# Attention windows with two expert layers on one core: opening order, input split by blocks, four weight stages

## The chip, the cores and the metric

One NeuronCore of a Trainium2 chip runs one program. The time is the device time of one execution in microseconds (us), lower is better. Engines: TensorE (PE), VectorE (DVE), ScalarE (ACT), GpSimd (POOL), and SyncE (SP), which issues every DMA of this kernel.

## The reference

Inputs r, k, v, w, a, b have the shape (4, 8, 768, 40), all float32. The recurrence over 768 tokens is, for each of 32 heads:

```
y[t]  = r[t] @ state
Sa    = state @ a[t]
state = state * w[t] - outer(Sa, b[t]) + outer(v[t], k[t])
```

y becomes x of (3072, 320). Then `h = ((x @ w1) * (x @ w2)) @ w3`, `x2 = h @ w_out`, with inner size 1024; then `g = max(x2 @ w_in, 0)`, `out = (g * g) @ w_out2`, with inner size 2048.

## The kernel before

**Attention.** The sequence is cut into 24 windows (n = 0 to 23) of 64 tokens of two batches. Each window goes through a fixed chain of steps on PE: `turn_w`, `turn_ar`, `turn_bk` (transposes of inputs), `cross`, `turn_rows`, `make_z`, then `make_u0`, `make_x1`, `make_u1` (a solve by blocks with inverted 32x32 blocks), `turn_uv`, `add_state`, `make_read`, `make_y`, `turn_state`. ACT and DVE stand between them: `scan`, `invert_decay`, `scale_a`, `scale_bk`, `mask_ak`, `fill_lanes`, `turn_inverse`, `add_x1`, `new_state`, `mask_read`, `scale_y` on DVE; `copy_r`, `copy_blocks`, `copy_rows`, `copy_x`, `reset`, `copy_u`, `copy_uvT`, `place_state`, `copy_state` on ACT. POOL computes the inverses (`invert`, L650 to L660): 31 steps of one multiplication and one addition per window, each step after the last; `turn_inverse(n)` on DVE hands the result to `make_u0(n)`. `store_y(n)` on SP writes y, transposed, to DRAM.

**Fold.** w3 @ w_out is multiplied out first, in eight row blocks `ft`: the block of w3 is loaded into a stage (`load_staged(ft)`), turned (`turn_w3`, PE), copied (`copy_w3`, ACT), multiplied in four quarters (`multiply_w3(ft, part)`, PE), split into a rounded high part and a rest (`round_fold` on ACT, `rest_of_fold` on DVE) and stored (`store_fold`, SP).

**Experts.** All large products run in a 4-byte type of lower precision, each operand being split in such a high part and a rest. The tokens go through in six tiles of 512; tile i needs windows 4i to 4i + 3, and `load_x`, `round_x` (ACT, the cast into `xT_hi`) and `rest_x` (DVE, `xT_lo`) bring its input. x has 320 rows, kept as three blocks of 128 (the last holds 64 rows twice, once for each of high part and rest). `into_hidden` (L854) multiplies a tile by one slice of w1, w2 or w_in with eight matmuls; `fold` (L907) and `project` (L922) multiply back. In the first tile each weight slice is split on the fly: SP loads it to a stage (`load_staged`), `round_split` (ACT) and `rest_of_split` (DVE) write it to a ring, `store_split` (SP) saves it to DRAM; later tiles load it from there. `splits` lists these slices in the order of their slots. There are LOOK = 3 stages; split x uses stage (8 + x) modulo 3, and `pass_split(x)` on SP stores split x and then loads x + 3.

**Order.** Each engine's program is a list written out by hand; semaphores connect the lists, and an engine does nothing past a step that waits. The opening is a flat list of steps: windows 0 to 3, the first part of windows 4 and 5, and the whole fold. Then come windows 4 to 23, whose steps are laced with those of the experts: after each step, `next(beside)` lets a generator do one piece of the experts. The first of these that PE does is `into_hidden("a0")` of tile 0, and `make_u0(4)` stands right behind it. Windows 0 to 3 use two PSUM areas (`both` for even n, `aside` for odd n), later ones `both` alone.

The lines that set the pace in what follows (before `make_u0`, and `turn_inverse` on DVE):

```
def make_u0(n):
    pe.wait_ge(inverse_turned, n + 1)
    pe.wait_ge(x_copied, n + 1)
    if n < OPENING - 1:
        pe.wait_ge(masked_ak, 2 * (n + 3))
        pe.wait_ge(blocks_copied, 2 * (n + 3))
```

Of the kernel before, what the change touches and what calls it, by code (L numbers as in the profile page):

```python
# [5 lines left out]
F32 = mybir.dt.float32  # L6
F32R = mybir.dt.float32r
ALU = mybir.AluOpType
# [69 lines left out]
def attention_with_experts(nc, xT_dram, inputs, w1, w2, w3, w_out, w_in, w_out2, out):  # L78
# [8 lines left out]
    T, M = out.shape  # L87
# [15 lines left out]
    LOOK = 3  # L103
# [10 lines left out]
    with ExitStack() as ctx:  # L114
# [33 lines left out]
        stage = [sb(f"stage{x}", [P, STAGE]) for x in range(LOOK)]  # L148
# [159 lines left out]

        staged_count = []
        for x in range(FT + len(splits)):  # L310
            before = staged_count[x - LOOK] if x >= LOOK else 0
            staged_count.append(before + 16 * (1 if x < FT or splits[x - FT][1] else 6))
# [9 lines left out]
        def staged_w(x):  # L322
            return stage[(FT + x) % LOOK][:, 0:2 * DX].rearrange("p (n c) -> p n c", n=2)

# [11 lines left out]
        def _(sp):  # L336
# [15 lines left out]
            def load_x(i, h):  # L352
                tile = xT_dram.rearrange("k (b s) -> k b s", b=B)[:, 2 * h:2 * h + 2, 2 * C * i:2 * C * (i + 1)]
                wait(sp, x_split, i)
# [15 lines left out]
            def load_staged(x):  # L370
                signal = staged[x % LOOK]
                if x < FT:
                    sp.dma_start(stage[x % LOOK][:], w3[x * P:(x + 1) * P, :]).then_inc(signal, 16)
                    return
                _, kind, at = splits[x - FT]
                if kind:
                    sp.dma_start(stage[x % LOOK][:, 0:M], w_out2[(at - FT) * P:(at - FT + 1) * P, :]).then_inc(signal, 16)
                    return
                for n in range(2):
# [5 lines left out]
                    for row in (0, REM):  # L385
                        sp.dma_start(dst[row:row + REM, 2 * P:DX], src[2 * P:M, lo:lo + P]).then_inc(signal, 16)
# [159 lines left out]
            next_staged(6)  # L546
            next_uv(2)
            next_ar(4)
            store_fold(2)
            next_staged(7)  # L550
            store_fold(3)
            store_y(0)
            next_bk(4)
            next_zv(4)
            next_w(5)
            next_uv(3)
            next_staged(8)
            next_ar(5)
            store_fold(4)
            store_y(1)  # L560
            next_bk(5)
            next_staged(9)
# [3 lines left out]
            store_fold(5)  # L566
            store_y(2)
            pass_split(0)
            load_x(0, 0)
            pass_split(1)  # L570
            store_y(3)
            load_x(0, 1)
            next_staged(10)
            store_fold(6)
# [96 lines left out]
        def _(pe):  # L671
# [198 lines left out]
            def turn_w3(ft):  # L870
                pe.wait_ge(staged[ft % LOOK], staged_count[ft])
                for part in range(PARTS):
                    u = PARTS * ft + part
                    wait(pe, w3_copied, u - 1)
                    for x in range(4):
                        g = 4 * part + x
                        last = nc.tensor.transpose(turning(u)[:, x * P:(x + 1) * P],
                                                   stage[ft % LOOK][:, g * P:(g + 1) * P], ident[:])
# [50 lines left out]
            def experts():  # L929
# [4 lines left out]
                for i in range(TILES):  # L934
# [6 lines left out]
                    pe.wait_ge(x_split, i + 1)  # L941
                    for f in range(FT + LAG):
                        if f < FT:
                            at = (FT + FT2 // 2) * i + f
                            wait_w(at)
                            for n, use in enumerate((f"a{f}", f"b{f}")):
                                wait_bank(pe, use, i)
                                into_hidden(use, w_ring[at % SLOTS], 5 * P * n, xT_hi, xT_lo)
# [66 lines left out]
            make_u0(1)  # L1015
            multiply_w3(4, 0)
            make_y(0)
            turn_state(0)
            make_x1(1)
            turn_rows(2)  # L1020
            multiply_w3(4, 1)
            make_u1(1)
            make_z(2)
            turn_uv(1)
            turn_w(4)
            multiply_w3(4, 2)
            add_state(1)
            turn_ar(4)
            multiply_w3(4, 3)
            make_read(1)  # L1030
            turn_bk(4)
            turn_w3(5)
# [4 lines left out]
            multiply_w3(5, 0)  # L1037
# [3 lines left out]
            make_x1(2)  # L1041
            multiply_w3(5, 1)
            turn_w3(6)
            make_u1(2)
            multiply_w3(5, 2)
            turn_uv(2)
            multiply_w3(5, 3)
            add_state(2)
            make_u0(3)
            make_read(2)  # L1050
            make_x1(3)
            make_y(2)
            turn_state(2)
            make_u1(3)
            turn_rows(4)
            turn_uv(3)
            make_z(4)
            add_state(3)
            multiply_w3(6, 0)
            make_read(3)  # L1060
            multiply_w3(6, 1)
            make_y(3)
            turn_state(3)
            multiply_w3(6, 2)
            turn_ar(5)
            multiply_w3(6, 3)
            turn_w3(7)
            turn_bk(5)
            multiply_w3(7, 0)
            cross(5)  # L1070
            multiply_w3(7, 1)
            multiply_w3(7, 2)
            multiply_w3(7, 3)
# [42 lines left out]
        def _(act):  # L1116
# [71 lines left out]
            def round_split(x):  # L1188
                _, kind, at = splits[x]
                act.wait_ge(staged[(FT + x) % LOOK], staged_count[FT + x])  # L1190
                if kind:
                    wait_slot_v(act, at)
                    nc.scalar.copy(v_ring[at % SLOTS][:, 0:M], stage[(FT + x) % LOOK][:, 0:M]).then_inc(v_rounded, 1)
# [24 lines left out]
            def round_x(i):  # L1218
# [3 lines left out]
                nc.scalar.copy(xT_hi[:], x_raw[:]).then_inc(x_rounded, 1)  # L1222
# [78 lines left out]
            place_state(0)  # L1301
            copy_u(1, 0, u0_made, u0_copied)
            copy_state(0)
            copy_rows(2)
            copy_u(1, 1, u1_made, u1_copied)
            copy_x(2)
            reset(2)
            copy_uvT(1)
            copy_r(4)
            place_state(1)  # L1310
            round_fold(4)
            copy_w3(5)
            copy_state(1)
            copy_blocks(4)
            copy_rows(3)
            copy_u(2, 0, u0_made, u0_copied)
            copy_x(3)
            reset(3)
            round_split(0)
            copy_w3(6)  # L1320
            copy_u(2, 1, u1_made, u1_copied)
            copy_uvT(2)
            round_fold(5)
            round_split(1)
            copy_u(3, 0, u0_made, u0_copied)
            place_state(2)
            copy_state(2)
            copy_u(3, 1, u1_made, u1_copied)
            copy_rows(4)
            copy_uvT(3)  # L1330
            copy_x(4)
# [3 lines left out]
            round_fold(6)  # L1335
            copy_w3(7)
            round_x(0)
            round_fold(7)
# [370 lines left out]
```

## Time and profile before

| | us |
|---|---|
| median of 3 runs | 1100.56 (1098.77 to 1101.25) |
| the profiled execution | 1100.62 |
| its span, first to last instruction | 1098.1 |
| PE busy | 1052.2 (96%) |
| DVE busy | 634.2 (58%) |
| ACT busy | 415.1 (38%) |
| POOL busy | 553.1 (50%) |

Mean granted clock of TensorE 0.984 of full speed. Busy time counts instructions on the engine, not DMA issues or waits. An engine that is idle is no loss by itself: it counts where the chain of work that ends last passes through it. DMA moved 172.74 MB.

### The profile page before, as it was taken

The numbers are of one execution on the slowest core, as the hardware profiler recorded it, in microseconds if no ns is written. First come the engines' busy times: TensorE is split into PE (matmuls) and PEld (weight loads), VectorE is DVE, ScalarE is ACT, GpSimd is POOL, SyncE is SP. The second block draws the span as 40 slices with busy tenths as digits, with TensorE's granted clock in tenths as the row PEclk, the third lists the DMA queues.
The fourth block names the chain that finished last, engine by engine and source line by source line (L and its number), as shares of the span: only waits on it lengthen the run. The fifth ranks groups of instructions, "written<-read, shape, count | busy, mean of one in ns | idle before, by whom it ended". The sixth has DMA issues, their size and how long they took to land.

```text
span 1098.1 us, 27872 instructions
## 1 busy us (share of the span) xinstructions
PE 1052.2 (96%) x11056; PEld 895.0 (81%) x11056; DVE 634.2 (58%) x987; ACT 415.1 (38%) x771; POOL 553.1 (50%) x1573
## 2 busy tenths in 40 slices
PE   6989689999989999999999999999999999999998
PEld 5767678778868888888888888888888888898897
DVE  7848256677757556656546657556566556333333
ACT  3444234344434234334234334224334234332232
POOL 4778727537555364585374575473675463600000
PEclk9999699999999999999999999999999999999999
DMA  9944367666768646647645658645557543546552
GB/s 169 190 101 92 84 182 201 157 170 188 190 201 229 148 135 150 151 147 196 158 138 136 151 154 204 156 130 141 148 160 202 146 136 103 156 144 227 180 166 76
DMA packets 269504, 172.74 MB, mean 157 GB/s; under 512 B 201792, under 2 KB 231488, under 8 KB 269376
## 3 DMA queue, kind: packets, MB, share of 16 engines
q1 hardware_dynamic: 269376, 170.97, 59.9%
q8 instruction: 88, 1.44, 0.6%
q14 instruction: 40, 0.33, 0.1%
HBM read 144.18 MB, written 26.74 MB: 156 GB/s over the span
## 4 chain that ended last, share of the span: by engine, by line
PE 77%; DVE 3%; issue 2%; SPq 2%; ACT 1%; DMA 0%; DVEq 0%; ACTq 0%
PE aside L854 30%; PE moe_bank L922 15%; PE moe_bank L907 9%; PE both L816 3%; PE both L717 3%; PE both L758 2%; PE both L750 2%; PE both L831 2%; PE both L827 2%; PE both L799 2%; PE both L701 1%; PE both L730 1%; PE both L840 1%; PE both L781 1%; PE both L807 1%
## 5 line engine op out<-in xcount | busy, mean ns | idle before, releaser
L656 POOL TENSOR_TENSOR inv_tmp<-blk,inv 128x60 f32<-128x60 f32 (+24 forms) x744 | 244.4, 328 | 252.2 <-DVE blk L1428 195.2
L660 POOL TENSOR_TENSOR inv<-inv,inv_tmp 128x60 f32<-128x60 f32 (+24 forms) x744 | 265.6, 357 | 58.3
L922 PE MATMUL moe_bank<-v_ring,h_hi 128*128 128x320 f32 x768 | 178.7, 320 | 0.0
L1508 DVE TENSOR_TENSOR hidden<-left 128x512 f32<-128x512 f32 x96 | 67.9, 707 | 129.6 <-ACT left L1216 129.6
L854 PE MATMUL aside<-xT_hi,w_ring 128*128 128x512 f32 x480 | 132.8, 406 | 0.1
L854 PE MATMUL aside<-x2T_hi,w_ring 128*128 128x512 f32 x480 | 132.7, 406 | 0.0
L922 PEld LDWEIGHTS moe_bank<-v_ring,h_hi 128*128 128x128 f32 x768 | 128.2, 190 | 3.3
L1496 DVE TENSOR_TENSOR h_lo<-hidden,h_hi 128x512 fp32r<-128x512 f32 x144 | 99.0, 688 | 48.1 <-ACT h_hi L1204 47.5
L1216 ACT ACTIVATE left<-aside 128x512 f32<-128x512 f32 x96 | 57.3, 597 | 172.2 <-PE aside L854 102.6
L922 PE MATMUL moe_bank<-v_ring,h_lo 128*128 128x320 f32 x384 | 119.2, 310 | 0.0
L1204 ACT CAST h_hi<-hidden 128x512 fp32r<-128x512 f32 x144 | 89.5, 621 | 77.0 <-DVE hidden L1504 38.4
L854 PEld LDWEIGHTS aside<-xT_hi,w_ring 128*128 128x128 f32 x480 | 84.5, 188 | 16.6 <-DVE xT_lo L1513 0.3
L854 PEld LDWEIGHTS aside<-x2T_hi,w_ring 128*128 128x128 f32 x480 | 84.1, 188 | 15.0 <-ACT x2T_hi L1242 0.2
L907 PE MATMUL moe_bank<-h_hi,v_ring 128*128 128x512 f32 x288 | 93.3, 405 | 0.0
L1386 DVE RECIPROCAL undecay<-decay 104x256 f32<-104x256 f32 x48 | 83.6, 1743 | 0.3
L854 PE MATMUL aside<-xT_lo,w_ring 128*128 128x512 f32 x288 | 81.5, 391 | 0.0
L854 PE MATMUL aside<-x2T_lo,w_ring 128*128 128x512 f32 x288 | 81.4, 391 | 0.0
L1504 DVE TENSOR_TENSOR hidden<-left,aside 128x512 f32<-128x512 f32 x48 | 32.8, 682 | 70.9 <-PE aside L854 70.9
L922 PEld LDWEIGHTS moe_bank<-v_ring,h_lo 128*128 128x128 f32 x384 | 72.8, 190 | 0.0
L854 PEld LDWEIGHTS aside<-x2T_lo,w_ring 128*128 128x128 f32 x288 | 54.1, 188 | 12.3 <-DVE x2T_lo L1532 0.2
L854 PEld LDWEIGHTS aside<-xT_lo,w_ring 128*128 128x128 f32 x288 | 54.1, 188 | 11.9
L1151 ACT COPY uv<-both 32x320 f32<-32x320 f32 x88 | 36.7, 417 | 62.2 <-PE both L758 60.8
(146 smaller groups left out, 1605.3 us busy)
## 6 DMA issues: line engine op xcount, KB each, us to landing
w_ring<-gate_rows SPq DMA_DIRECT2D x40, 640.0 KB, 4.6
w_ring<-win_rows SPq DMA_DIRECT2D x40, 640.0 KB, 4.1
v_ring<-wout_rows SPq DMA_DIRECT2D x80, 320.0 KB, 3.0
v_ring<-fold_rows SPq DMA_DIRECT2D x48, 384.0 KB, 4.1
gate_rows<-w_ring SPq DMA_DIRECT2D x8, 640.0 KB, 3.8
win_rows<-w_ring SPq DMA_DIRECT2D x8, 640.0 KB, 4.1
wout_rows<-v_ring SPq DMA_DIRECT2D x16, 320.0 KB, 2.8
stage<-in_moe_w SPq DMA_DIRECT2D x8, 512.0 KB, 4.9
```

The source lines that it names most:

```text
L656: nc.gpsimd.tensor_tensor(tmp, x[:, j, 0:j].unsqueeze(2).broadcast_to([P, j, X - lo]), mine[:, j:j + 1, lo:X].broadcast_to([P, j, X - lo]) ...
L660: nc.gpsimd.tensor_tensor(mine[:, 0:j, lo:X], mine[:, 0:j, lo:X], tmp, ALU.add).then_inc(solve, 1)
L717: last = nc.tensor.matmul(its_both(n)[:, x * P:(x + 1) * P], bkT[n % 2][0:E, x].rearrange("e z s -> e (z s)"), azk[n % 2][0:E, x].rearrang ...
L854: last = nc.tensor.matmul(bank(use), w, x, start=n == 0, stop=n == len(terms) - 1)
L907: last = nc.tensor.matmul(bank(f"x{m}"), weights[:, lo:lo + P], h[at % RING][:], start=f == 0 and n == 0, stop=f == FT - 1 and n == 2)
L922: last = nc.tensor.matmul(bank(f"o{s}")[:, 0:M], h[at % RING][:, s * P:(s + 1) * P], weights[:, rest * M:(rest + 1) * M], start=f == 0 and ...
L1151: last = nc.scalar.copy(uv[n % 2][rows, :, q, 0:D], by_head(its_first(n), rows))
L1204: nc.scalar.copy(h_hi[at % RING][:], hidden[x % 2][:]).then_inc(hi_made, 1)
L1216: drain(nc.scalar.activation(left[x % 2][:], bank(use), ACT.Relu), use)
L1386: nc.vector.reciprocal(undecay[0:E, xs], decay[n % 4][0:E, xs, 1:C + 1]).then_inc(undecayed, 1)
L1496: nc.vector.tensor_tensor(h_lo[at % RING][:], hidden[x % 2][:], h_hi[at % RING][:].bitcast(F32), ALU.subtract).then_inc(lo_made, 1)
L1508: nc.vector.tensor_tensor(hidden[x % 2][:], left[x % 2][:], left[x % 2][:], ALU.mult).then_inc(squared, 1)
```

## The change

Three things. First, `LOOK` is 4: a fourth stage, only as large as a weight slice. w3's blocks go on using the stages 0 to 2; the slices use 3, 2, 0, 1 in turn. `pass_split(x)` loads x + 4, and the opening loads four slices (8 to 11) by `next_staged`. The last 64 rows of a slice, which go to the stage twice, are loaded by one DMA whose source is repeated, where there were two DMAs; a slice thus takes four DMAs, not six.

Second, `round_x` and `rest_x` do a tile's input in three blocks, and the matmuls of `into_hidden("a0")` wait for the block that each reads, not for the whole.

Third, the lists of the opening are laid out anew on all engines but POOL. Nothing is added or left out.

```diff
-    LOOK = 3
+    LOOK = 4
-        stage = [sb(f"stage{x}", [P, STAGE]) for x in range(LOOK)]
+        stage = [sb(f"stage{x}", [P, STAGE if x < LOOK - 1 else 2 * DX]) for x in range(LOOK)]
...
+        def stage_of(x):
+            return x % (LOOK - 1) if x < FT else (3, 2, 0, 1)[(x - FT) % LOOK]
...
-                    for row in (0, REM):
-                        sp.dma_start(dst[row:row + REM, 2 * P:DX], src[2 * P:M, lo:lo + P]).then_inc(signal, 16)
+                    twice = src[2 * P:M, lo:lo + P].unsqueeze(0).broadcast_to([2, REM, P])
+                    sp.dma_start(dst[:, 2 * P:DX], twice).then_inc(signal, 16)
...
             def next_staged(x):
-                sp.wait_ge(turned_w3, PARTS * (x - LOOK + 1))
+                before = [y for y in range(min(x, FT)) if stage_of(y) == stage_of(x)]
+                wait(sp, turned_w3, PARTS * (before[-1] + 1) if before else 0)
...
-                    pe.wait_ge(x_split, i + 1)
+                    def wait_x(n):
+                        if n in (0, 2, 4):
+                            pe.wait_ge(x_rounded, 3 * i + n // 2 + 1)
+                        elif n > 4:
+                            pe.wait_ge(x_split, 3 * i + n - 4)
...
-                nc.scalar.copy(xT_hi[:], x_raw[:]).then_inc(x_rounded, 1)
+                for k in range(3):
+                    nc.scalar.copy(xT_hi[:, k], x_raw[:, k]).then_inc(x_rounded, 1)
...
-                dve.wait_ge(x_rounded, i + 1)
-                nc.vector.tensor_tensor(xT_lo[:], x_raw[:], xT_hi[:].bitcast(F32), ALU.subtract).then_inc(x_split, 1)
+                for k in range(3):
+                    dve.wait_ge(x_rounded, 3 * i + k + 1)
+                    nc.vector.tensor_tensor(xT_lo[:, k], x_raw[:, k], xT_hi[:, k].bitcast(F32),
+                                            ALU.subtract).then_inc(x_split, 1)
```

The new lists from `turn_w3(4)` on (m(ft, part) is `multiply_w3`):

```
PE    turn_w3(4) make_read(0) m(4,0) turn_w3(5) make_y(0) turn_state(0) make_u0(1) turn_rows(2) make_x1(1)
      make_z(2) turn_w(4) make_u1(1) m(4,1) turn_uv(1) turn_ar(4) add_state(1) m(4,2) make_read(1) turn_bk(4)
      make_y(1) turn_state(1) cross(4) turn_rows(3) m(4,3) make_u0(2) turn_w(5) make_z(3) make_x1(2) m(5,0)
      make_u1(2) m(5,1) turn_uv(2) m(5,2) add_state(2) m(5,3) make_read(2) turn_w3(6) make_y(2) turn_state(2)
      m(6,0) turn_rows(4) m(6,1) make_u0(3) make_z(4) make_x1(3) m(6,2) make_u1(3) m(6,3) turn_uv(3)
      turn_w3(7) add_state(3) m(7,0) make_read(3) m(7,1) make_y(3) turn_state(3) m(7,2) turn_ar(5) m(7,3)
      turn_bk(5) cross(5)
ACT   copy_w3(4) place_state(0) copy_w3(5) copy_state(0) copy_u(1,0) copy_rows(2) round_split(0) copy_x(2)
      reset(2) copy_u(1,1) copy_uvT(1) copy_r(4) place_state(1) copy_state(1) copy_blocks(4) copy_rows(3)
      round_fold(4) copy_u(2,0) copy_x(3) reset(3) copy_u(2,1) copy_uvT(2) place_state(2) round_fold(5)
      copy_w3(6) copy_state(2) copy_rows(4) copy_u(3,0) round_split(1) copy_x(4) copy_u(3,1) round_fold(6)
      copy_uvT(3) copy_w3(7) place_state(3) copy_state(3) copy_r(5) round_fold(7) round_x(0)
DVE   new_state(0) rest_of_fold(3) mask_read(0) turn_inverse(1) fill_lanes(3) scale_y(0) add_x1(1)
      rest_of_split(0) scan(4) invert_decay(4,0) invert_decay(4,1) new_state(1) scale_a(4) mask_read(1)
      scale_bk(4) scale_y(1) turn_inverse(2) mask_ak(4) fill_lanes(4) scan(5) add_x1(2) rest_of_fold(4)
      invert_decay(5,0) invert_decay(5,1) new_state(2) rest_of_fold(5) mask_read(2) scale_y(2)
      turn_inverse(3) add_x1(3) rest_of_split(1) rest_of_fold(6) new_state(3) mask_read(3) scale_y(3)
      scale_a(5) rest_of_fold(7) scale_bk(5) rest_x(0)
```

The old list of PE in the same part, where it differs most: `... turn_w3(4) make_read(0) make_u0(1) m(4,0) make_y(0) ...`, then `... m(5,3) add_state(2) make_u0(3) make_read(2) make_x1(3) make_y(2) turn_state(2) make_u1(3) turn_rows(4) turn_uv(3) make_z(4) add_state(3) m(6,0) make_read(3) m(6,1) make_y(3) turn_state(3) m(6,2) turn_ar(5) m(6,3) turn_w3(7) turn_bk(5) m(7,0) cross(5) m(7,1) m(7,2) m(7,3)`.

## Rows read from the trace of the kernel before

**Rows 1.** The page's 40 slices: PE's busy tenths and its clock in tenths.
```profile
PE   6989689999989999999999999999999999999998
PEclk9999699999999999999999999999999999999999
```

**Rows 2.** Timeline of PE, 0 to 200 us: start, duration, instructions, [idle before, releaser].
```profile
69.24 1.06 PE L758 MATMUL aside<-x_row,invT 32*32 32x40 f32 x32 [3.73 <-DVE invT L1434]
...
97.74 0.76 PE L758 MATMUL both<-x_row,invT 32*32 32x40 f32 x32 [0.76 <-DVE azk L1419]
98.43 0.65 PE L685 MATMUL both<-ident,w_raw 64*104 64x64 f32 x8
...
107.28 1.24 PE L889 MATMUL moe_bank<-wo_raw,hidden 128*128 128x320 f32 x4
108.54 0.81 PE L807 MATMUL both<-uv,bk_row 128*40 128x40 f32 x32
118.21 1.28 PE L758 MATMUL aside<-x_row,invT 32*32 32x40 f32 x32 [8.85 <-DVE invT L1434]
...
135.13 0.81 PE L807 MATMUL aside<-uv,bk_row 128*40 128x40 f32 x32
...
137.05 1.95 PE L816 MATMUL aside<-rbd,uvT 104*128 104x128 f32 x16
...
149.46 2.05 PE L717 MATMUL both<-azk,bkT 104*128 104x128 f32 x16 [0.24 <-DVE bkT L1407]
...
158.95 0.76 PE L758 MATMUL both<-x_row,invT 32*32 32x40 f32 x32 [2.28 <-DVE azk L1419]
```

**Rows 3.** Waits of PE, 160 us to the end: total, times, longest; first of five.
```profile
PE both L799 <- DVE decay L1378: 5.2, 1, 5.2
...
```

**Rows 4.** Timeline of POOL: copies that start inverses, and one long step.
```profile
68.43 0.40 POOL L650 COPY inv<-inv_unit 128x256 f32<-128x256 f32 x1
...
91.97 0.40 POOL L650 COPY inv<-inv_unit 128x256 f32<-128x256 f32 x1
...
103.85 2.26 POOL L656 TENSOR_TENSOR inv_tmp<-blk,inv 128x64 f32<-128x64 f32 x1
...
117.39 0.40 POOL L650 COPY inv<-inv_unit 128x256 f32<-128x256 f32 x1
```

**Rows 5.** Stretches of PE: from:to, length, busy (count), granted clock, DMA share, GB/s.
```profile
128.00:131.00 3.00, 3.00 (x72) 0.50 0.20 45
...
310.00:312.00 2.00, 2.00 (x11) 0.53 0.92 327
```

**Rows 6.** Timeline of DVE, 0 to 215 us.
```profile
96.08 1.41 DVE L1419 TENSOR_TENSOR azk<-both,above 64x512 f32<-64x512 f32 x2
...
103.67 1.75 DVE L1386 RECIPROCAL undecay<-decay 104x256 f32<-104x256 f32 x1
105.34 0.63 DVE L1488 TENSOR_TENSOR w_ring<-stage,w_ring 128x512 fp32r<-128x512 f32 x1
...
142.48 0.69 DVE L1470 TENSOR_TENSOR y_out<-aside,decay 104x512 f32<-104x512 f32 x1 [2.22 <-PE aside L831]
...
152.57 1.76 DVE L1513 TENSOR_TENSOR xT_lo<-x_raw,xT_hi 128x1536 fp32r<-128x1536 f32 x1 [3.17 <-ACT xT_hi L1222]
...
155.65 0.73 DVE L1434 STREAM_TRANSPOSE invT<-inv 128x256 f32<-128x256 f32 x1
```

**Rows 7.** Timeline of ACT, at 151 and at 305 us.
```profile
151.07 1.47 ACT L1222 CAST xT_hi<-x_raw 128x1536 fp32r<-128x1536 f32 x1 [3.07 <-DMA x_raw<-xT]
...
304.68 0.83 ACT L1196 CAST w_ring<-stage 128x768 fp32r<-128x768 f32 x1 [4.86 <-DMA stage<-in_moe_w_in]
```

**Rows 8.** Timeline of SP's DMA issues, 268 to 330 us.
```profile
287.81 0.62 SPq L399 DMA_DIRECT2D wout_rows<-v_ring  x1
...
296.14 0.47 SPq L383 DMA_DIRECT2D stage<-in_moe_w_in  x1
```

**Rows 9.** DMA queue, 104.6 to 109.3 us, one slice's load: packets, MB, share.
```profile
q1 hardware_dynamic: 784, 0.36, 27.2%
```

More of the change, by code:

```diff
@@ L307, in due @@
             return [x for x, (slot, _, _) in enumerate(splits) if x >= EARLY and slot == t - LEAD]
+        def stage_of(x):
+            return x % (LOOK - 1) if x < FT else (3, 2, 0, 1)[(x - FT) % LOOK]
         staged_count = []
         for x in range(FT + len(splits)):
-            before = staged_count[x - LOOK] if x >= LOOK else 0
-            staged_count.append(before + 16 * (1 if x < FT or splits[x - FT][1] else 6))
+            counted = [staged_count[y] for y in range(x) if stage_of(y) == stage_of(x)]
+            staged_count.append((counted or [0])[-1] + 16 * (1 if x < FT or splits[x - FT][1] else 4))
         clears = [azk[0], rbd[0], azk[1], rbd[1], *spare, *zv, *sT, *st]
@@ L1014, in _ @@
             make_read(0)
-            make_u0(1)
             multiply_w3(4, 0)
+            turn_w3(5)
             make_y(0)
             turn_state(0)
+            make_u0(1)
+            turn_rows(2)
             make_x1(1)
-            turn_rows(2)
+            make_z(2)
+            turn_w(4)
+            make_u1(1)
             multiply_w3(4, 1)
-            make_u1(1)
-            make_z(2)
             turn_uv(1)
-            turn_w(4)
+            turn_ar(4)
+            add_state(1)
             multiply_w3(4, 2)
-            add_state(1)
-            turn_ar(4)
-            multiply_w3(4, 3)
             make_read(1)
             turn_bk(4)
-            turn_w3(5)
             make_y(1)
@@ L1036, in _ @@
             turn_rows(3)
-            multiply_w3(5, 0)
+            multiply_w3(4, 3)
             make_u0(2)
@@ L1041, in _ @@
             make_x1(2)
+            multiply_w3(5, 0)
+            make_u1(2)
             multiply_w3(5, 1)
-            turn_w3(6)
[L1044 to L1051, printed above, removed]
+            turn_uv(2)
+            multiply_w3(5, 2)
+            add_state(2)
+            multiply_w3(5, 3)
+            make_read(2)
+            turn_w3(6)
             make_y(2)
             turn_state(2)
+            multiply_w3(6, 0)
+            turn_rows(4)
+            multiply_w3(6, 1)
+            make_u0(3)
+            make_z(4)
+            make_x1(3)
+            multiply_w3(6, 2)
             make_u1(3)
-            turn_rows(4)
+            multiply_w3(6, 3)
             turn_uv(3)
-            make_z(4)
+            turn_w3(7)
             add_state(3)
-            multiply_w3(6, 0)
+            multiply_w3(7, 0)
             make_read(3)
-            multiply_w3(6, 1)
+            multiply_w3(7, 1)
             make_y(3)
             turn_state(3)
-            multiply_w3(6, 2)
+            multiply_w3(7, 2)
             turn_ar(5)
-            multiply_w3(6, 3)
-            turn_w3(7)
+            multiply_w3(7, 3)
             turn_bk(5)
-            multiply_w3(7, 0)
             cross(5)
-            multiply_w3(7, 1)
-            multiply_w3(7, 2)
-            multiply_w3(7, 3)
             for n in range(OPENING, WINDOWS):
@@ L1315, in _ @@
             copy_rows(3)
+            round_fold(4)
             copy_u(2, 0, u0_made, u0_copied)
@@ L1602, in _ @@
             new_state(0)
+            rest_of_fold(3)
+            mask_read(0)
             turn_inverse(1)
             fill_lanes(3)
-            mask_read(0)
-            rest_of_fold(3)
             scale_y(0)
             add_x1(1)
+            rest_of_split(0)
             scan(4)
             invert_decay(4, 0)
+            invert_decay(4, 1)
             new_state(1)
             scale_a(4)
-            invert_decay(4, 1)
             mask_read(1)
             scale_bk(4)
+            scale_y(1)
             turn_inverse(2)
-            rest_of_fold(4)
-            scale_y(1)
             mask_ak(4)
@@ L1621, in _ @@
             scan(5)
+            add_x1(2)
+            rest_of_fold(4)
             invert_decay(5, 0)
-            add_x1(2)
             invert_decay(5, 1)
-            rest_of_split(0)
+            new_state(2)
             rest_of_fold(5)
-            new_state(2)
+            mask_read(2)
+            scale_y(2)
             turn_inverse(3)
+            add_x1(3)
             rest_of_split(1)
-            mask_read(2)
-            add_x1(3)
-            scale_y(2)
+            rest_of_fold(6)
             new_state(3)
```

70 lines of the change are left out of this document (35 added, 35 removed).

## The prediction

> **What bounds the kernel now.** I read the slices of the page first, then TensorE's order of time, then the list of its waits, and last the engines that those name. The slices [rows 1] show TensorE (PE) at 9 tenths nearly everywhere; the weak ones lie in the first 15% of the span, and the granted clock dips there too. Later PE is busy without pause. So a microsecond taken out of an early wait of PE comes off the end; one taken off another engine later is worth nothing. The waits of PE worth naming [rows 2, 3]: 3.73 us before `make_u0(1)` at 69.24, 8.85 us before `make_u0(3)` at 118.21, 2.28 us before `make_u0(4)` at 158.95, and one of 5.2 us in the experts' first tile (before `turn_uv`, at 309 us). The first two are waits for an inverse: POOL works on them back to back, one from 68.43 to 91.97 (23.54 us), the next to 117.39 (25.42) [rows 4]. During the 8.85 us PE still has `make_read(2)`, `make_y(2)`, `turn_state(2)` and the last two of W3's eight row blocks to do, but they stand behind `make_u0(3)` in its queue. After that wait the clock is low, 0.50 (1.2 GHz) still in 128 to 131 [rows 5]; `make_read(3)` at 137.05 takes 1.95 us again.
>
> **Opening, up to the third inverse.** The new order puts `turn_w3(5)`, `make_y(0)` and `turn_state(0)` ahead of `make_u0(1)`, so PE is busy on from 65.5 (69.24 - 3.73). From 69.24 to 97.74 the old order took 28.5 us [rows 2]; about 3.8 of it were small waits and low clock, and it had one quarter of a `multiply_w3` (1.24) more than the new one has there. That gives 65.5 + 28.5 - 3.8 - 1.2 = 89.0, and 90.5 with two waits that I find in the new order (`turn_rows(2)` for `scale_y(0)`, `turn_uv(1)` for `copy_u(1, 1)`, which has moved behind `reset(2)`). There PE waits: `make_u0(2)` needs `mask_ak(4)`, which is behind `turn_inverse(2)` on DVE, and this waits for POOL until 91.97: + 0.8 to turn it + 2.3 for the mask (1.41 [rows 6] and two copies) gives 95.0, against 97.74. The new wait, 4.5 us, holds up all that is behind it on PE, but not the path: from there to the end of `add_state(2)` the old order took 11.6 us (97.74 to 109.35 [rows 2]). With `make_read(2)` 1.95, its mask 1.2, `make_y(2)` 2.0, `turn_state(2)` 0.8, `turn_rows(4)` 0.9 and two quarters of W3 at 1.1 a piece, PE arrives at `make_u0(3)` at 115.7. The inverse is later still.
>
> **When inverse 3 ends.** Its 25.42 us hold one TENSOR_TENSOR of 2.26 us at 103.85 [rows 4], where its neighbours take 0.3. It ran beside DVE's reciprocal at 103.67, right behind which stood `rest_of_split(0)` (from 105.34 [rows 6]), and ended in the middle of that. The new order has no such pair there: `rest_of_split(0)` comes at some 74.5 us. So I take 23.5 us as for inverse 2, and 0.5 for what `rest_of_split(0)` now costs inverse 2: 91.97 + 0.5 + 23.5 = 116.0, and 0.82 on to `make_u0(3)` (117.39 to 118.21): **T0 = 116.9**. With a 2.26 us op again it is 118.9.
> The Trainium skill (SBUF — State Buffer, "SBUF: two separate sides") lets a DVE op with two SBUF inputs shut out POOL's reads, but names nothing by which a reciprocal would; by it the cause of the first 1.5 us is another and may stay, T0 would be 118.4 and the time 1082.9.
>
> **From T0 to the experts.** Window 2 shows the same chain at full clock: `make_u0` at 97.74 to `add_state` at 108.54, 10.80 us [rows 2]. The new one for window 3 lacks `turn_w` (0.6) and two quarters of W3 (2.3): 7.9. Then `add_state` to `make_read`, 1.92 (135.13 to 137.05); to the end of `scale_y(3)`, 6.12 (143.17 [rows 6]); y's way through DRAM to the cast of x, 7.90 (ACT at 151.07 [rows 7]). Sum: ACT begins `round_x(0)` at T0 + 23.8. PE's own way there, ending in `cross(5)`, ended 8.3 us after `scale_y(3)` before (149.46 + 2.05 = 151.51); now with one quarter of W3 less in front, 7.2: hidden by x, by little.
> Split by blocks: one cast of 1.47 and one subtraction of 1.76 [rows 6, 7] become three each, of 0.6 by estimate (a third, and 0.1 for an instruction more); a subtraction starts 0.65 after its cast, and the last ends 2.4 us after ACT began, against 3.26. PE may begin 0.65 us after ACT, not 3.5. But behind the eight matmuls of `a0` stands `make_u0(4)`, which needs `mask_ak(5)`, behind `rest_x(0)` on DVE: 3.30 us from `turn_inverse(4)` to it (155.65 to 158.95), and `rest_of_fold(7)` is gone from between them. So it comes at ACT + 5.7, where it was + 7.88. The split is worth 2.2 us, not the 2.9 that PE gains at the door; its wait before `make_u0(4)` grows from 2.28 to 2.8. In the five later tiles x is ready long before and no wait of PE is for it [rows 3], so it is worth 0 there, and the 0.3 us more on ACT and on DVE lie beside PE's matmuls.
> `make_u0(4)` at 116.9 + 23.8 + 5.7 = 146.4, was 158.95: **12.5 us**. With T0 = 118.9 it is 10.5, with 0.6 less of small waits 13.1.
>
> **Four stages, not three.** The 5.2 us at 309 go back so: `turn_uv` waits for DVE's scan; this stands behind `rest_of_split` of a w_in slice, and that behind ACT's cast, which sat idle 4.86 us until its stage had landed, at 304.68 [rows 7]. SP issued that load only from 296.14 on, six issues to 300.9. With four stages it goes out one split earlier, behind the store at 287.81 [rows 8], and with four issues is out at 291.5; landed at 294 to 297. ACT is free for it at 299.8. So the wait goes whole, and the scan's input (`turn_w`, done at 301.0) is no later than the old one's slot. It also takes the low clock behind it (0.53 in 310 to 312 [rows 5]): 3 us at half speed, 1.5. Together **6.7 us**, bounds 0 (late all the same) and 7.5. No other cast waits for a stage, so the other early loads bring 0, and two issues less of 0.57 us a slice only relieve SP.
> One DMA where two were: its source repeats 64 rows twice, the repeat outermost. In the old trace the 784 packets of one slice took 27.2% of 16 engines over 4.7 us [rows 9], 0.026 us each. Spread over 16 engines, nothing changes. Should only two engines carry the 128 packets, two such transfers a slice put 6.7 us on two engines together, 3.3 each if they share, up to 6.7 if not, and the slice lands 3 us later, at 297 to 300: still in time for 299.8. I take 6.7 either way.
> The Trainium skill speaks for the bad case (DMA: Bandwidth & Descriptors, "Rules for kernel authors": an outermost zero-stride dim of c copies confines the DMA to c engines); no row here shows which engine carries what.
>
> **Sum.** The profiled execution took 1100.6 (span 1098.1), the runs' median to 0.1. 1100.6 - 12.5 - 6.7 = **1081.4 us**; own range 1078 to 1085.
>
> **Rivals.**
> (a) The clock. After 8.85 us of waiting PE ran at half speed for some 15 us. If the 4.5 us before `make_u0(2)`, or the short waits around T0, bring that on in the tail, which holds some 15 us of PE's work, 7.5 us come back: 1088.9. For it: after the 3.73 us `make_u0(1)` took 1.06 for 0.76. Against: by the later rows this was over soon. 14%.
> (b) The stage's load is late again, SP's queue having shifted with all the rest: 1100.6 - 12.5 = 1088.1. Against: 3 to 5 us of margin. 9%.
> (c) The other side: two engines carry the repeated rows, and what is queued behind them on these (window inputs, ring loads) comes late. Twelve slices are loaded in the first tile, each with 2.9 us more (3.3 for 0.4) on either engine; if PE waits for all of it, 35 us: 1116. It turns the sign from 1.6 us a slice on (19.2 / 12). For it: DMA is half to nine tenths busy in that stretch. Against: no wait in [rows 3] is for a DMA. 4%.
> (d) The order stalls where I overlooked something and the two cancel, within 0.2% (2.2 us, what can be told from no change here): 3%.
> The forecast has 70%. Faster 0.94, same 0.03, slower 0.03 (a part of (c) only eats the gain). Range for 8 in 10: 1077 to 1088.5.
>
> **What would show it.** PE without a gap from 62 to 70; a wait of 4 to 5 us before `make_u0(2)` near 95; `make_u0(3)` at 116 to 118 with PE there first; the first expert matmul near 141.5, `make_u0(4)` near 146; no idle ACT for `stage` in the first tile, and no wait of PE at `turn_uv` there. A `make_u0(3)` before 115 would refute that POOL sets it; a time over 1086 means a low clock or a late load.

## The result, and the profile after

The changed kernel takes 1083.82 us (median of 6 runs, 1081.31 to 1085.83) against 1100.6 (6 runs, 1098.37 to 1102.04): a ratio of 0.9849 [0.9829, 0.9869], so 1.5% faster. A later group of 6 runs of the same changed kernel (`e9_after_again`) gave 1086.18, 1.2% faster than the old kernel beside it. The forecast was 1081.4, in a range from 1077 to 1088.5. The execution with the profile took 1085.12 us, its span 1082.9 (before 1098.1).

The page's slices, which answer to [rows 1]: the 6 of the busy share and the 6 of the clock, both in the fifth slice (110 to 137 us), have gone. The clock now dips twice, to 8 tenths, in the fourth slice (81 to 108 us) and in the sixth (135 to 162).

```profile
PE   6998989999999999999999999999999999999998
PEclk9998989999999999999999999999999999999999
```

TensorE's timeline of the changed kernel, 60 to 300 us, against [rows 2]; the bracket is the idle time before a row and what released it. L764 is `make_u0` and `make_u1`, L723 `cross`, L805 `turn_uv`; `make_u0(2)` is at 95.94, `make_u0(3)` at 118.34, `make_u0(4)` at 147.96, `make_u0(5)` at 159.98.

```profile
69.91 0.81 PE L846 MATMUL both<-ident,sT 40*40 40x40 f32 x32
70.65 0.76 PE L764 MATMUL aside<-x_row,invT 32*32 32x40 f32 x32
...
90.39 1.26 PE L895 MATMUL moe_bank<-wo_raw,hidden 128*128 128x320 f32 x4
...
95.94 0.88 PE L764 MATMUL both<-x_row,invT 32*32 32x40 f32 x32 [4.29 <-DVE azk L1432]
...
99.63 1.28 PE L787 MATMUL both<-uv,n 32*32 32x40 f32 x32
...
118.34 0.76 PE L764 MATMUL aside<-x_row,invT 32*32 32x40 f32 x32
...
140.22 3.27 PE L723 MATMUL both<-azk,bkT 104*128 104x128 f32 x16 [1.32 <-DVE bkT L1420]
143.14 1.90 PE L860 MATMUL aside<-xT_hi,w_ring 128*128 128x512 f32 x5
...
147.96 1.28 PE L764 MATMUL both<-x_row,invT 32*32 32x40 f32 x32 [2.22 <-DVE azk L1432]
...
159.98 0.76 PE L764 MATMUL both<-x_row,invT 32*32 32x40 f32 x32 [0.33 <-DVE x_row L1454]
...
295.36 1.05 PE L805 MATMUL both<-ident,uv 128*104 128x128 f32 x8 [1.12 <-DVE decay L1391]
```

The 3.73 us before `make_u0(1)` and the 8.85 before `make_u0(3)` have no successor there. A new wait of 4.29 us stands before `make_u0(2)`. The 5.2 us before `turn_uv` in the first expert tile are 1.12, and its eight transposes take 1.05 us. In the old trace they took 1.92:

```profile
308.96 1.92 PE L799 MATMUL both<-ident,uv 128*104 128x128 f32 x8 [5.20 <-DVE decay L1378]
```

Stretches of TensorE behind the waits of the opening (from:to, length, busy (count), granted clock, DMA share, GB/s):

```profile
96.00:99.00 3.00, 3.00 (x64) 0.58 0.02 5
99.00:102.00 3.00, 3.00 (x48) 0.50 0.00 0
102.00:105.00 3.00, 3.00 (x39) 0.79 0.41 132
...
141.00:144.00 3.00, 3.00 (x14) 0.50 0.43 123
...
147.00:150.00 3.00, 2.04 (x34) 0.61 1.10 346
150.00:153.00 3.00, 3.00 (x9) 0.50 0.80 172
153.00:156.00 3.00, 3.00 (x16) 0.75 1.28 197
```

After the 4.29 us and after the 2.22 us the clock is at 0.50, its 1.2 GHz level, for some 7 us each, and for some 3 us behind the 1.32 us before `cross(5)`, whose 16 matmuls took 3.27 us where the old trace has 2.05. This last one lies off the path, since `make_u0(4)` waits for DVE's mask behind it. What the old trace had low behind `turn_uv`, at 310 us, is at full clock.

**Where the 15.2 us of span come from**, by the starts of the same steps in both traces: 11.0 at `make_u0(4)` (158.95 to 147.96). 3.0 of it are lost again by `make_u0(5)`: 12.02 us between the two, where the old trace has 9.05 (168.0 - 158.95). 1.5 come from a low clock that the old execution had behind a 1.7 us wait at 242 us, and the new one not behind its own at 234. 4.1 are the wait before `turn_uv`, and 1.6 the low clock behind that. 11.0 - 3.0 + 1.5 + 4.1 + 1.6 = 15.2.

The other engines. POOL's copies that start an inverse, against [rows 4]:

```profile
68.56 0.40 POOL L656 COPY inv<-inv_unit 128x256 f32<-128x256 f32 x1
...
92.61 0.40 POOL L656 COPY inv<-inv_unit 128x256 f32<-128x256 f32 x1
...
116.04 0.40 POOL L656 COPY inv<-inv_unit 128x256 f32<-128x256 f32 x1
```

Inverse 3 takes 23.43 us and has no step over 0.81; the 2.26 us step is gone. Its end at 116.04 is the forecast 116.0. ACT (the first split x block, against [rows 7], and the only cast of the first tile that waits for a stage), and DVE (the first subtraction of a block):

```profile
142.21 1.66 ACT L1235 CAST xT_hi<-x_raw 128x512 fp32r<-128x512 f32 x3 [4.29 <-DMA x_raw<-xT]
...
292.64 0.46 ACT L1205 CAST v_ring<-stage 128x320 fp32r<-128x320 f32 x1 [1.61 <-DMA stage<-in_moe_w_out]
```
```profile
142.86 1.90 DVE L1527 TENSOR_TENSOR xT_lo<-x_raw,xT_hi 128x512 fp32r<-128x512 f32 x3 [2.69 <-ACT xT_hi L1235]
```

SP's issues, against [rows 8]:

```profile
276.29 0.43 SPq L387 DMA_DIRECT2D stage<-in_moe_w_in  x1
...
286.33 0.47 SPq L381 DMA_DIRECT2D stage<-in_moe_w_out  x1
```

The w_in slice that was late is now issued at 276.29 and its cast (at 290.20) waits for nothing. Late is the next slice, one of w_out, issued at 286.33 behind a ring store: ACT waits 1.61 us for it, DVE's split waits 0.54 for ACT, and the scan that `turn_uv` needs stands behind that.

### The profile page after: what moved, and what is told of

Same layout as the page of the kernel before. It is cut to its first block, busy times and chain, and to the rows that moved or that the text cites. A ratio compares the mean times of both kernels' runs of the same rounds, so it can differ in the third digit from the quotient of the medians.

```text
span 1082.9 us, 27864 instructions
## 1 busy us (share of the span) xinstructions
PE 1048.2 (97%) x11056; PEld 890.9 (82%) x11056; DVE 635.4 (59%) x999; ACT 416.7 (38%) x783; POOL 552.2 (51%) x1573
## 4 chain that ended last, share of the span: by engine, by line
PE 77%; DVE 3%; issue 3%; SPq 1%; ACT 1%; DMA 1%; DVEq 0%; ACTq 0%
PE aside L860 30%; PE moe_bank L928 15%; PE moe_bank L913 9%; PE both L822 3%; PE both L723 3%; PE both L764 2%; PE both L756 2%; PE both L837 2%; PE both L833 2%; PE both L805 2%; PE both L736 1%; PE both L707 1%; PE both L813 1%; PE both L846 1%; PE both L787 1%
## 5 line engine op out<-in xcount | busy, mean ns | idle before, releaser
L928 PEld LDWEIGHTS moe_bank<-v_ring,h_lo 128*128 128x128 f32 x384 | 72.1, 188 | 0.0
```

The lines of the kernel that those rows point to most:

```text
L928: last = nc.tensor.matmul(bank(f"o{s}")[:, 0:M], h[at % RING][:, s * P:(s + 1) * P], weights[:, rest * M:(rest + 1) * M], start=f == 0 and ...
```

## The experiments

Each had 4 to 6 timed runs. The changed kernel itself was timed in two groups, in its first measurement (1083.82) and as a control in a later group (1086.18, `e9_after_again`): medians of the same program differ by 2.4 us between groups, so a microsecond or two is told only inside one group, and where the time went is read from the traces, segment by segment. All segments below are differences of rows of the timelines (us; A: `make_u0(0)`; B: `make_u0(0)` to `(3)`; C: `(3)` to `(4)`; D: `(4)` to `(5)`; E: `(5)` to that `turn_uv` in the first expert tile and, bracketed, the wait in front of it; F: from there to the end):

| kernel | A | B | C | D | E | F | median |
|---|---|---|---|---|---|---|---|
| before | 48.41 | 69.80 | 40.74 | 9.05 | 140.96 (5.20) | 789.1 | 1100.6 |
| after | 49.15 | 69.19 | 29.62 | 12.02 | 135.38 (1.12) | 787.5 | 1083.8 |
| e1 three stages | 51.45 | 69.52 | 29.86 | 9.04 | 140.45 (4.81) | 789.0 | 1091.3 |
| e2 stages only | 51.31 | 68.21 | 40.00 | 9.30 | 134.84 (0.64) | 787.9 | 1093.9 |
| e3 two DMAs | 51.38 | 68.75 | 29.94 | 12.30 | 136.52 (2.29) | 788.9 | 1089.7 |
| e4 x whole | 48.81 | 72.06 | 31.20 | 11.30 | 138.87 (3.05) | 787.8 | 1088.5 |
| e5 mask first | 49.07 | 67.38 | 34.43 | 12.07 | 134.89 (0.65) | 787.5 | 1087.7 |
| e6 kept busy | 51.05 | 69.55 | 29.51 | 9.04 | 137.86 (2.04) | 787.4 | 1087.4 |
| e7 first wait too | 50.91 | 67.08 | 28.92 | 9.05 | 138.02 (2.26) | 787.4 | 1083.1 |
| e8 both | 50.87 | 66.96 | 28.63 | 9.03 | 139.32 (3.54) | 788.9 | 1085.4 |
| e9 after again | 50.78 | 70.00 | 29.22 | 9.05 | 136.45 (0.63) | 787.7 | 1086.2 |
| e10 load first | 51.40 | 66.33 | 33.03 | 9.05 | 138.45 (2.63) | 787.4 | 1082.6 |
| e11 e7 again | 51.19 | 66.67 | 33.78 | 9.02 | 138.05 (3.83) | 789.0 | 1085.2 |

Groups run together: e1 to e4; e5, e6; e7 to e9; e10, e11. A is the same order in all but before and e2, and varies by 2.6 us (48.81 to 51.45). E without its wait is 134.2 or 135.8, F 787.4 to 787.9 or 788.9 to 789.1: a low clock behind a wait near 235 us, and behind the one at `turn_uv`, that falls or doesn't. What sets A is open. All spans stand 1.7 to 2.5 us under their own execution's time.

**e1: the change without the fourth stage.**
```diff
-    LOOK = 4
+    LOOK = 3
...
-        stage = [sb(f"stage{x}", [P, STAGE if x < LOOK - 1 else 2 * DX]) for x in range(LOOK)]
+        stage = [sb(f"stage{x}", [P, STAGE]) for x in range(LOOK)]
...
-                    twice = src[2 * P:M, lo:lo + P].unsqueeze(0).broadcast_to([2, REM, P])
-                    sp.dma_start(dst[:, 2 * P:DX], twice).then_inc(signal, 16)
+                    for row in (0, REM):
+                        sp.dma_start(dst[row:row + REM, 2 * P:DX], src[2 * P:M, lo:lo + P]).then_inc(signal, 16)
```


> The change without its fourth stage: new order and input by blocks, three stages, six DMAs a slice. Theory (the stages give what the two traces show, 4.1 us of the wait before turn_uv and 1.2 of low clock): the wait of some 5 us before turn_uv near 300 us is back, opening as in the changed kernel (make_u0(4) near 148), 1089 us. Rival (the wait is a matter of how SP's queue falls, and the new order alone would have moved it away): no wait above 2 us there, 1084 us.

1091.32 us (1090.47 to 1091.62), 0.9917 [0.9903, 0.9932]. The wait is back and with it the late stage. TensorE in e1:
```profile
300.32 1.92 PE L804 MATMUL both<-ident,uv 128*104 128x128 f32 x8 [4.81 <-DVE decay L1390]
```
ACT in e1:
```profile
296.02 0.83 ACT L1207 CAST w_ring<-stage 128x768 fp32r<-128x768 f32 x1 [4.45 <-DMA stage<-in_moe_w_in]
```
E and F together are 6.6 above the changed kernel's, but 1.4 of it is the low clock at 242 us (E without its wait: 135.64, 134.26). The stages' share is 3.7 of wait and 1.5 of low clock behind it: 5.2. That share is of two executions: with four stages the wait is 0.63 to 3.83 us from one to the next, with three it is 4.81 here and 5.20 before. The medians differ by 5.1 to 7.5. C is not touched.

**e2: the old kernel with the fourth stage and the repeated source only.** The same lines as in e1, the other way round, and one `next_staged(11)` in SP's opening.
```diff
-    LOOK = 3
+    LOOK = 4
...
-                    for row in (0, REM):
-                        sp.dma_start(dst[row:row + REM, 2 * P:DX], src[2 * P:M, lo:lo + P]).then_inc(signal, 16)
+                    twice = src[2 * P:M, lo:lo + P].unsqueeze(0).broadcast_to([2, REM, P])
+                    sp.dma_start(dst[:, 2 * P:DX], twice).then_inc(signal, 16)
```


> The kernel before with the fourth stage and four DMAs a slice alone. Theory: make_u0(4) at 159 as before, the 5.2 us wait before turn_uv down to about 1.1, ACT idle for a stage at most 2 us: 1095 us. Rival (two engines carry the repeated rows and delay what is behind them): a new wait elsewhere in the first tile, 1098 us or more.

1093.85 us (1092.28 to 1095.78), 0.9942 [0.9927, 0.9957]: 7.0 under the old kernel of its group (1100.85). E and F are 7.3 shorter than before, 1.5 of it at 242 us, so 5.8 by the stages. The opening (C 40.00, and a wait of 9.91 us before `make_u0(3)`) is as it was. With the old order POOL's long step is there too:
```profile
105.03 2.17 POOL L662 TENSOR_TENSOR inv_tmp<-blk,inv 128x64 f32<-128x64 f32 x1
```
So it goes with the order, not with the stages.
In this trace one slice's load stands alone, issued until 103.7. The stretches behind, in e2 (columns as above):
```profile
105.00:106.00 1.00, 1.00 (x34) 1.00 0.14 41
106.00:107.00 1.00, 1.00 (x8) 1.00 0.20 56
107.00:108.00 1.00, 1.00 (x9) 1.00 0.01 4
```
It trickles for 3.5 us behind the last issue. In the old trace the last issue ends at 108.64 and the last packet at 109.8. That is what few engines would show, and rival (c)'s premise: by the Trainium skill (DMA: Bandwidth & Descriptors, "Rules for kernel authors") an outermost zero stride of two copies confines the transfer to at most two engines, and the tail agrees. No row names an engine. The price that rival (c) put on it did not come: no wait of TensorE in the first tile names a DMA.

**e3: the changed kernel with the repeated rows by two DMAs.** My theory after the result: the 1.12 us left before `turn_uv` come from the slow repeated load. The rival: from SP, which issues it late.
```diff
-                    twice = src[2 * P:M, lo:lo + P].unsqueeze(0).broadcast_to([2, REM, P])
-                    sp.dma_start(dst[:, 2 * P:DX], twice).then_inc(signal, 16)
+                    for row in (0, REM):
+                        sp.dma_start(dst[row:row + REM, 2 * P:DX], src[2 * P:M, lo:lo + P]).then_inc(signal, 16)
```


> The changed kernel with the last 64 rows of a slice loaded by two DMAs again, six a slice. Theory (the source whose outer dimension is a repeat of two is carried by few engines, and the 1.6 us for which ACT waits for a w_out stage near 292 us comes from there): these DMAs land some 2.5 us after issue, that wait of ACT and the 1.1 us of PE behind it go, 1082.5 us. Rival (SP's issues are the limit there, two more per slice make it worse): PE waits 2 us or more there, 1085 us.

1089.74 us (1089.28 to 1090.19), 0.9904 [0.9886, 0.9921]. The two waits did not go. ACT in e3:
```profile
296.17 0.46 ACT L1205 CAST v_ring<-stage 128x320 fp32r<-128x320 f32 x1 [2.76 <-DMA stage<-in_moe_w_out]
```
My theory fell: with the plain transfers the same slice is late. That two issues more a slice make it later is not shown. With the repeated source in place ACT waits 0.15 to 4.32 us for it in the executions of e2 and e4 to e11, and TensorE 0.63 to 3.83 before `turn_uv`; the 2.76 and 2.29 us here lie inside both. All four runs lie above all six of the changed kernel's first measurement, but in another group, and the later group of the changed kernel reaches 1090.49. 2.2 us of the profiled difference are A, which the edit does not touch.

**e4: x in one piece.**
```diff
-                for k in range(3):
-                    nc.scalar.copy(xT_hi[:, k], x_raw[:, k]).then_inc(x_rounded, 1)
+                nc.scalar.copy(xT_hi[:], x_raw[:]).then_inc(x_rounded, 1)
...
-                    dve.wait_ge(x_rounded, 3 * i + k + 1)
...
+                dve.wait_ge(x_rounded, i + 1)
...
+                    pe.wait_ge(x_split, i + 1)
...
```


> The changed kernel with the input of a tile rounded and split in one piece again. Theory: ACT begins at the same 142.2, make_u0(4) comes 2.2 us later (near 150.2), and since PE is the limit from there on the time is 1086 us. Rival (the split is worth nothing, as make_u0(4) waits for the mask anyway, or the clock falls the same way in both): 1084 us.

1088.49 us (1085.19 to 1091.82), 0.9895 [0.9877, 0.9912]. TensorE in e4, the first expert matmul:
```profile
148.38 2.47 PE L860 MATMUL aside<-xT_hi,w_ring 128*128 128x512 f32 x5 [2.44 <-DVE xT_lo L1519]
...
152.07 1.28 PE L764 MATMUL both<-x_row,invT 32*32 32x40 f32 x32
```
`make_u0(4)` comes 7.21 us after ACT's first cast of x (at 144.86), against 5.75 in the changed kernel: 1.5 us, where I had 2.2. Half of it is the clock. `make_u0(4)` has no wait here: the eight expert matmuls in front of it ran at 1.2 GHz (3.7 us for e9's 2.3) and ended at 152.07, when DVE's mask had been ready since 151.02. With the 0.25 us that lie between mask and `make_u0(4)` in the changed kernel, it would have come at 151.3, and the split would be worth 0.7 us. Later tiles do not show the split (F 787.8 against 787.5 and 787.7). B is 72.06, the longest of all, in a part that the edit does not touch: the clock was at 0.50 for some 14 us behind the first wait, where the changed kernel has 7.

**e5: the mask ahead of the inverse's turn on DVE.** Theory: the 4.29 us and the half clock behind them cost what T0 is late, and `mask_ak(4)` needs no inverse.
```diff
             scale_y(1)
-            turn_inverse(2)
             mask_ak(4)
+            turn_inverse(2)
             fill_lanes(4)
```


> The changed kernel with mask_ak(4) ahead of turn_inverse(2) on DVE. Theory (PE's 4.3 us wait before make_u0(2) is the mask's place in DVE's list; it is long enough to drop the clock to half until 103, and this is why PE, not POOL, is last at make_u0(3)): the wait shrinks to about 2 us, the clock stays full, make_u0(3) at 116.9 where POOL sets it, 1.4 us less: 1082.4 us. Rival (the clock falls after a 2 us wait as well): make_u0(3) at 118 or later, 1084 us.

1087.68 us (1085.0 to 1089.19), 0.9875 [0.9854, 0.9895], a miss: 1082.4 was expected. TensorE's timeline in e5:
```profile
93.01 0.76 PE L764 MATMUL both<-x_row,invT 32*32 32x40 f32 x32 [1.72 <-DVE invT L1447]
...
116.45 1.23 PE L764 MATMUL aside<-x_row,invT 32*32 32x40 f32 x32 [3.98 <-DVE invT L1447]
```
and its stretches:
```profile
117.00:120.00 3.00, 3.00 (x69) 0.50 0.15 36
120.00:123.00 3.00, 3.00 (x28) 0.50 0.45 126
```
`make_u0(3)` is 1.9 us earlier (B 67.38, POOL sets it) but the wait has moved there, and the half clock with it, to where it is on the path: C grows by 4.8. A wait in front of a point that another engine sets can't be removed, only placed.

**e6: work for TensorE in the tail's waits.** 39 transposes whose result nobody reads, in front of the steps that wait: 4, 11, 6 and 18.
```diff
+            def keep_busy(count):
+                for _ in range(count):
+                    nc.tensor.transpose(banks[2][:, 0:P], ident[:], ident[:])
...
+            keep_busy(11)
             cross(5)
```


> The changed kernel with 39 transposes that nobody reads put into PE's waits at the end of the opening: 4 before turn_bk(5), 11 before cross(5), 6 before the first expert matmul, 18 before make_u0(4), sized to the waits of the trace. Theory (the half clock from 141 to 154 us costs 3 us and comes from these waits): the clock stays full there, make_u0(4) to make_u0(5) takes 9.1 us instead of 12.0, and the time is 1081 us, every run near it. Rival (the clock falls for another reason, or the transposes take more than they give): 1084 to 1086 us.

1087.41 us (1083.9 to 1089.3), 0.9875 [0.985, 0.99]. D is 9.04, as the theory wanted, but so it is in the control e9 without a transpose; to `make_u0(5)` the two are within 0.1 us (159.15, 159.05). No gain in time is shown. What the transposes do for the clock shows over all executions: from `cross(5)` to `make_u0(5)` it stayed full in the five that have them (e6, e7, e8, e10, e11; D is 9.02 to 9.05) and fell in five of the six of the new order that have not (after, e1, e3, e4, e5, not in e9).

**e7, e8 and the control e9.** e7 is e6 with 34 transposes before `make_u0(2)`, set to run when W3's part is copied. e8 has e5's order with 24 before `make_u0(3)`. e9 is the changed kernel, not edited.
```diff
             multiply_w3(4, 3)
+            pe.wait_ge(w3_copied, PARTS * 6)
+            keep_busy(34)
             make_u0(2)
```


> The changed kernel with unread transposes in all of PE's long waits: the 39 of before at the end of the opening and 34 more before make_u0(2) (4.3 us of waiting, 3.7 us of transposes). Theory (half clock after waits is what the forecast missed: 1.4 us at make_u0(3), 3.0 us behind make_u0(4)): clock 1.0 from 90 to 155, make_u0(3) 20.9 us after make_u0(2), i.e. at 116.8 where POOL sets it, make_u0(4) 29.6 later, make_u0(5) 9.05 after that; 4.4 us less than the changed kernel measured beside it. Rival (the clock falls whatever stands in the waits): no gain over it.

> The changed kernel with mask_ak(4) ahead of turn_inverse(2), 24 unread transposes before make_u0(3) and the 39 at the end of the opening. Theory (moving the mask only moved PE's wait to make_u0(3), where the low clock falls on the path; filled, nothing is lost): make_u0(3) at 116.5, 67.4 us after make_u0(0), make_u0(4) 29.6 us later and make_u0(5) 9.05 later, time as the first of these three or 0.3 us better, 4.5 us below the changed kernel beside it. Rival (POOL's inverse is later for the mask's place): make_u0(3) 1 us later, 3.5 us.

> The changed kernel as it is, beside the other two on one chip, since profiled executions of one order differ by 2 us before the first window's solve and by 1.5 us behind the wait of 1.7 us near 234. Theory (these two are chance of the clock, not of the kernel): the time is 1083 to 1087 us, so 3 to 4 us above the other two; runs spread by 4 us. Rival (the first six runs were typical, the experiments slower by what they changed): 1083.8 within 0.5.

e7 1083.1 us (1080.2 to 1085.73), 0.9848 [0.9822, 0.9873]; e8 1085.44 (1081.57 to 1086.59), 0.9857 [0.9831, 0.9882]; e9 1086.18 (1083.88 to 1090.49), 0.9881 [0.9855, 0.9907]. e7 is 3.1 below the control in the medians, with intervals that overlap; 4.4 was expected. e8 is 0.7 below it, for an expected 4.5: a miss in time, though its B and C (66.96, 28.63) came as the theory had them. e7's stretches, against 0.58 and 0.50 above:
```profile
93.00:96.00 3.00, 3.00 (x30) 1.00 0.44 74
...
99.00:102.00 3.00, 3.00 (x79) 1.00 0.02 5
```
and its `make_u0(3)`:
```profile
117.99 0.76 PE L764 MATMUL aside<-x_row,invT 32*32 32x40 f32 x32 [1.68 <-DVE invT L1458]
```
The clock stays, TensorE comes first and waits for the inverse. B is 66.3 to 67.1 in the four executions with transposes before `make_u0(2)` or `make_u0(3)` (e7, e8, e10, e11), and 67.4 in e5, where the mask is moved. It is 68.8 to 72.1 in the six that leave the first wait empty and in place (after, e1, e3, e4, e6, e9), where the clock is at 0.50 for 7 to 14 us behind it. In their own group e7 and e8 are 2.9 and 3.0 us below the control e9: the price of the low clock behind that wait.

**e10 and the control e11.** e10 is e7 with a slice's load issued ahead of the ring store; e11 is e7, not edited.
```diff
             def pass_split(x):
-                store_split(x)
+                _, kind, at = splits[x]
+                sp.wait_ge(v_split if kind else w_split, at - FT + 1 if kind else at + 1)
                 if x + LOOK < len(splits):
                     load_staged(FT + x + LOOK)
+                store_split(x)
```


> The kernel with all waits of PE filled (e7_first_wait_too), and pass_split(x) on SP now issues the load of slice x + 4 ahead of the store of slice x, where it came behind it. Theory (what is left of the wait before turn_uv in the first tile, 0.6 to 3.5 us, is the w_out slice's load issued behind a 640 KB store and landing 6 us later in a stretch where DMA moves 400 GB/s): ACT waits for that stage under 1 us, PE under 0.5, and 1 to 2 us are gone against e7_first_wait_too beside it. Rival (the DMA is full there, and the order of issues changes nothing): the same wait, the same time.

> The kernel of e7_first_wait_too as it was, beside the other: 1080 to 1086 us, median near 1083, wait before turn_uv between 0.6 and 3.5 us.

e10 1082.58 us (1079.19 to 1087.4), 0.9849 [0.9822, 0.9877]; e11 1085.22 (1083.85 to 1089.38), 0.9864 [0.9838, 0.989]. The wait before `turn_uv` is 2.63 and 3.83 and not gone, so the store in front of the load is not the whole cause; the times do not tell the two apart. The rival of e10's expectation, that the DMA is full there, fits: the load went out at 289.44, ahead of the store, and landed at 295.49, some 6 us later, as in the changed kernel (286.33 to 292.64). There the DMA engines were busy all the time before it landed (from:to, length, clock, DMA share, GB/s):
```profile
290.00:292.00 2.00, 1.00 1.03 403
```
Both profiled executions have 4 us more in C than e7. The clock fell right behind the wait before `make_u0(3)`, which none of e7, e10 and e11 fills (only e8 has transposes there), and was full again before the filled waits of the tail. TensorE in e10, where e7 took 1.34 us for the second row:
```profile
117.73 0.76 PE L766 MATMUL aside<-x_row,invT 32*32 32x40 f32 x32 [1.34 <-DVE invT L1460]
...
120.84 2.50 PE L897 MATMUL moe_bank<-wo_raw,hidden 128*128 128x320 f32 x4
```
e11 fell behind 1.68 us of the same wait, e7 did not behind its 1.68. The best of these, e7 and e10, cannot be told from the changed kernel's first measurement.

## Why the prediction was right

**The places held, and the size nearly; the sum was 2.4 us too good by the first measurement and 4.8 by the second.** Step by step:

- TensorE arrives before `make_u0(2)` at 90.5 and waits 4.5 us, to 95.0. Measured: the last row before ends at 91.65 (90.39 + 1.26), the wait is 4.29, the step at 95.94. Of the 1.15 us by which TensorE arrives late, 0.74 are the start A; of the 0.94 by which the wait ends late, 0.64 are the inverse, which ends at 92.61 for 91.97.
- The inverse ends at 116.0 because the 2.26 us step goes. Measured 116.04. Both kernels with the old order have the step, the one with the new has not; no run put DVE's pair of operations alone back, so that it is the cause is not shown. The estimate worked from the Trainium skill (SBUF — State Buffer, "SBUF: two separate sides"), that 1.5 us of it may stay, did not come true here.
- T0, set by POOL, at 116.9. Measured 118.34: this is **the step that failed**. The sum gave TensorE full clock behind the 4.5 us wait and had it at `make_u0(3)` at 115.7. It ran at 1.2 GHz for 6 us, came 2.6 us late, and POOL had been done for 2.3. e7 shows the other case: clock 1.00, and the wait for POOL's inverse is there. Rival (a) named this wait, but priced only the tail.
- T0 to `make_u0(4)`: forecast 29.5, measured 29.62, and the wait there 2.8 against 2.22. Inside it x's way through DRAM took 8.09 us (134.12 to 142.21) for 7.90. Two things in this term came out right by luck. First, the 7.9 us from `make_u0(3)` to `add_state(3)` (measured 7.74) rest on window 2 "at full clock", and the old trace has that chain at 0.50 around 102 us. One quarter of W3 took 2.50 us there, about twice its time at full clock:
```profile
101.16 2.50 PE L889 MATMUL moe_bank<-wo_raw,left 128*128 128x320 f32 x4
```
  That left some 1.5 us too much in the term (1.1 there and 0.4 in the step before it). Against it, the new order lacks one quarter of W3 there (three in the old trace, two in the new) and not two, 1.1 us. Second, the 2.2 us put down to the split hold two causes. In the old trace DVE began `turn_inverse(4)` 3.08 us after `rest_x(0)` (152.57 to 155.65), with `rest_of_fold(7)` between them; in e4, which has x whole and the new order, 1.67 (146.37 to 148.04). So 1.4 us come from the order and 0.7 from the split.
- Behind `make_u0(4)` the sum had nothing. The profiled execution lost 3.0 us there to the low clock. In other executions it did not: C + D is 37.7 to 38.9 us in five (e1, e6 to e9) and 41.6 to 42.8 in four (after, e3, e10, e11): in the first two of these the clock fell at `make_u0(4)`, where no transposes stand, in the last two behind the unfilled wait before `make_u0(3)`. So rival (a)'s mechanism is there, at 3 to 5 us for its 7.5 and by turns; what decides between two executions with the same wait is open.
- The fourth stage: forecast 6.7. Measured 4.1 + 1.6 = 5.7 in the profile, 5.2 by e1's trace, 5.8 by e2's. The waiting w_in slice is in time, as forecast; "goes whole" failed by what is late next, the w_out slice behind it, for 0.6 to 3.8 us from execution to execution.
- The repeated source: both cases were priced at nothing. e3 does not speak against it, as its waits lie inside the spread of the others.
- Of the signs named beforehand, the wait near 95 and the gapless stretch from 62 to 70 us came. `make_u0(3)` at 118.34 with POOL there first, the first expert matmul at 143.14 (141.5 was forecast), an ACT that waits 1.61 us for a stage and the 1.12 us at `turn_uv` did not fit.

12.5 + 6.7 = 19.2 was forecast; the profile has 11.0 - 3.0 + 5.7 + 1.5 = 15.2, where the 1.5 at 242 us is no gain of the change: e1, e4, e6 to e10 have it too (E without its wait 135.6 to 135.8), and e2, e3, e5 and e11 not (134.2), with the edits on either side. The runs' medians differ by 16.8, since the profiled execution is one of the slower three of six. That the first measurement lies nearer to 1081.4 than the second is luck too.

## What to carry to other kernels

When a reordering takes a wait off the critical path, ask where TensorE will wait instead, and charge for the steps behind that wait at half clock: here 4.3 us of waiting off the path made the next point on it 1.4 us later than POOL alone would. A wait in front of a step that another engine paces can be moved, not removed, so place it where most slack follows it; and for a buffer made deeper, look one transfer further on for the one that becomes the late one. Before a microsecond is given a cause, look at the same segment in two executions of one kernel: here single segments differed by 3 to 5 us without any edit.

## What was not expected of the hardware

- The clock fell behind waits as short as 1.3 us (before `cross(5)` in the changed kernel, before `make_u0(3)` in e10). It fell behind 2.2 us at `make_u0(4)` in one execution and stayed behind 2.62 us there in another (e9, D 9.05); behind a 1.7 us wait near 235 us it fell in some executions and not in others, for 1.5 us. Such pieces of 1.5 to 4 us are of the size of a single kernel's spread, up to 8 us: e10's profiled execution had a mean clock of 0.990 and took 1087.4, another one 0.998 and 1079.19.
- 34 transposes in the first wait kept the clock at 1.00 through 102 us, and 39 in the tail's waits kept it there in all five executions that have them. In e10 and e11 it fell earlier, behind 1.34 and 1.68 us that were left empty.
- One load with its source repeated trickled at 41 to 56 GB/s for some 3.5 us, and still two plain transfers in its place, with two SP issues more a slice, showed no gain.
